# Products with w_in by Strassen's seven multiplications, and layer one for all tokens before layer two

## What is computed

```python
def _moe_ref(x, w_in, w_out, s, b):
    h = x @ w_in
    r = np.maximum(h, 0.0)
    g = s * (r * r) + b
    return g @ w_out

def _moe2_ref(x, w_in, w_out, alpha):
    h = x @ w_in
    g = np.maximum(h, 0.0) + alpha * np.minimum(h, 0.0)
    return g @ w_out
```

## Time and profile before

| | |
|---|---|
| median of 3 timed runs | 1099.71 us (1098.87 to 1099.93) |
| span of the profiled execution | 1098.9 us; nothing shows its own time apart from that |
| matmuls | 4867, of which 4608 in the steps |
| TensorE busy (PE) | 1086.0 us |
| VectorE busy (DVE) | 635.3 us |
| ScalarE busy (ACT) | 592.0 us |
| GpSimd busy (POOL) | 14.6 us |
| moved by DMA | 33.44 MB |

### The profile page before, as it was taken

How to read it: one execution, slowest core, us unless ns; L and a number is a source line. 1 busy time by engine, 2 the same in 40 slices (tenths; PEclk the granted TensorE clock), 3 DMA queues, 4 the chain that set the end, 5 groups by cost and what they waited for, 6 DMA issues and landing times.

```text
span 1098.9 us, 14358 instructions
## 1 busy us (share of the span) xinstructions
PE 1086.0 (99%) x4867; PEld 909.9 (83%) x4867; DVE 635.3 (58%) x980; ACT 592.0 (54%) x1073; POOL 14.6 (1%) x19
## 2 busy tenths in 40 slices
PE   8899999999999999999999999999999999999998
PEld 6788888888888888888888888888888888889887
DVE  6877755645645645655555555564564564565554
ACT  5565646446546546545545644644654654654654
POOL 1110000000000000000000000000000000000000
PEclk9999999999999999999999999999999999999999
DMA  9632201101101001011010010110110000001010
GB/s 356 228 96 77 58 1 20 20 1 20 20 0 19 7 12 19 0 19 19 0 19 15 4 19 0 19 19 0 19 19 0 14 7 12 1 1 20 1 20 16
DMA packets 106719, 33.44 MB, mean 30 GB/s; under 512 B 98480, under 2 KB 103104, under 8 KB 106176
## 3 DMA queue, kind: packets, MB, share of 16 engines
q1 hardware_dynamic: 106560, 33.04, 12.0%
q0 software_dynamic: 128, 0.01, 0.0%
HBM read 26.88 MB, written 6.16 MB: 30 GB/s over the span
## 4 chain that ended last, share of the span: by engine, by line
PE 98%; DMA 1%; DVE 0%; SPq 0%; ACT 0%; issue 0%; DVEq 0%
PE acc L375 16%; PE hid L375 16%; PE acc L377 16%; PE hid L377 16%; PE acc L376 16%; PE hid L376 16%; PE acc L438 4%; DMA qk_raw<-in_k_dram 1%; PE hid L480 0%; PE hid L485 0%; PE hid L481 0%; SPq L289 0%; PE acc L480 0%; PE acc L481 0%; PE acc L485 0%; DVE logit L754 0%
## 5 line engine op out<-in xcount | busy, mean ns | idle before, releaser
L555 ACT ACTIVATE pos<-hid 128x512 f32<-128x512 f32 (+1 forms) x384 | 225.3, 587 | 265.0 <-PE hid L377 263.2
L375 PE MATMUL acc<-act_hi,wo_hi 128*128 128x512 f32 (+1 forms) x768 | 295.5, 385 | 0.0
L377 PE MATMUL acc<-act_hi,wo_lo 128*128 128x512 f32 (+1 forms) x768 | 295.3, 385 | 0.0
L376 PE MATMUL acc<-act_lo,wo_hi 128*128 128x512 f32 (+1 forms) x768 | 295.3, 385 | 0.0
L700 DVE SCALAR_TENSOR_TENSOR act<-neg,nalpha,pos 128x512 f32<-128x512 f32 (+1 forms) x192 | 142.2, 741 | 235.0 <-ACT pos L555 235.0
L678 DVE TENSOR_TENSOR act_lo<-act,act_hi 128x512 fp32r<-128x512 f32 (+1 forms) x384 | 258.4, 673 | 0.1
L697 DVE TENSOR_TENSOR act<-pos 128x512 f32<-128x512 f32 (+1 forms) x192 | 130.4, 679 | 200.9 <-ACT pos L555 199.5
L533 ACT ACTIVATE act_hi<-act 128x512 fp32r<-128x512 f32 (+1 forms) x384 | 237.8, 619 | 0.3 <-DVE act L700 0.3
L554 ACT ACTIVATE neg<-hid 128x512 f32<-128x512 f32 (+1 forms) x192 | 113.2, 589 | 203.9 <-PE hid L377 203.9
L375 PEld LDWEIGHTS acc<-act_hi,wo_hi 128*128 128x128 f32 x768 | 144.2, 188 | 27.9 <-DVE act_lo L678 0.5
L376 PEld LDWEIGHTS acc<-act_lo,wo_hi 128*128 128x128 f32 x768 | 144.2, 188 | 27.4
(11 more groups left out here) (101 smaller groups left out, 556.1 us busy)
## 6 DMA issues: line engine op xcount, KB each, us to landing
v_raw<-in_v_dram SPq DMA_DIRECT2D x44, 128.0 KB, 3.3
out_dram<-y_sq SPq DMA_DIRECT2D x44, 128.0 KB, 2.5
qk_raw<-in_q_dram SPq DMA_DIRECT2D x10, 512.0 KB, 11.2
qk_raw<-in_k_dram SPq DMA_DIRECT2D x10, 512.0 KB, 12.2
stage<-in_moe_w_in_dram SPq DMA_DIRECT2D x4, 1024.0 KB, 9.1
stage<-in_moe_w_out_dram SPq DMA_DIRECT2D x4, 1024.0 KB, 5.4
qk_raw<-in_q_dram SPq DMA_DIRECT2D x1, 384.0 KB, 12.1
qk_raw<-in_k_dram SPq DMA_DIRECT2D x1, 384.0 KB, 13.5
```

What stands on the lines that cost most here:

```text
L375: pe.matmul(dst, w_hi, x_hi, start=start, stop=False)
L376: pe.matmul(dst, w_hi, x_lo, start=False, stop=False)
L377: return pe.matmul(dst, w_lo, x_hi, start=False, stop=stop)
L555: sc.activation(pos[:, f % 2, 0:w], hid[:, f % 2, 0:w], ACT.Relu).then_inc(relu_done, 1)
```

## The change

Tokens now go in pairs of tiles, five pairs of 2 x 512 and one of 2 x 448. For a pair, hidden units (two halves of 1024), channels (two blocks of 128) and tokens (two tiles) make a 2 x 2 by 2 x 2 product of blocks, and that is made by Winograd's form of Strassen's scheme: seven products in place of eight. One of 8 steps j handles 128 units of either half, that is four blocks of hidden (C11, C12, C21, C22).

- Weights: `ws_hi` and `ws_lo` hold for each j the four blocks of w_in and the sums S1 to S4 in seven slots. For layer one DVE (first half) and POOL (second half) make the sums before the steps; for layer two POOL makes them during the last pair of layer one, and ACT and DVE split them then (`ws_high`, `ws_low`, `wo_high`, `wo_low`: the swap, steps 40 to 49 of 96). Only one layer's weights lie in SBUF.
- Tokens: POOL makes the four sums of a pair's blocks (`x_sums`) and all seven low parts (`x_low`), ACT the seven high parts (`x_high`), during the pair before.
- PE makes seven products a step into four banks, three of them accumulating onto an earlier one. ACT copies product 1 out of PSUM (`copy_m1`), DVE adds it up with others (`sum_u2`, `sum_u3`, `sum_c22`, `sum_c21`, `sum_c12`); C11 is a bank of PSUM as it stands. Then relu, gate and split as before, layer one's squares of C22 and C11 on ACT. `project` is unchanged in number: 24 matmuls a step.
- Layer one runs for all six pairs and stores its output to `x2_dram` in DRAM; then layer two loads it (`load_x`) pair by pair. A pair's output goes through three slots `ev`.
- Everything is unrolled. q and k have 7 load slots in place of 8.

The core of the diff:

```diff
+TILE = 512
+PAIRS = 6
+LAST_TILE = (N - (PAIRS - 1) * 2 * TILE) // 2
+STEPS = NF // 2
+PROD = 7
+RUNS = 2 * PAIRS
...
+A11, S2, S3, S1, A12, A22, S4 = range(PROD)
+
+C11, C12, C21, C22 = range(4)
+
+X_ORDER = (0, 4, 6, 1, 3, 2, 5)
...
+    x2_dram = nc.dram_tensor("x2_dram", (PAIRS, 2, CB, P, TILE), F32, kind="Internal").ap()
...
+        SWAP = (PAIRS - 1) * STEPS
+
+        def ws_step(i):
+
+            return i // 2 if i < STEPS else SWAP + i - STEPS + 1
+
+        def wo_step(i):
+            return i - 1 if i < STEPS else SWAP + i - STEPS + 2
...
+            for run in range(RUNS):
+                for j in range(STEPS):
+                    n = run * STEPS + j
+                    if j == 0 and run + 1 < PAIRS:
+                        load_v(run + 1, 0)
+                    if j == 0 and PAIRS <= run + 1 < RUNS:
+                        load_x(run + 1)
+                    if run == 0 and j + 2 < STEPS:
+                        load_wo(j + 2)
+                    if n in (SWAP, SWAP + 1):
+                        load_wo(STEPS + n - SWAP)
+                    if 3 <= n - SWAP <= STEPS:
+                        load_wo(STEPS + n - SWAP - 1)
+                    if 0 <= n - SWAP < STEPS:
+                        load_w2(n - SWAP)
+                    if j == 0 and run > 0:
+                        for t in range(2):
+                            for b in range(CB):
+                                store(run - 1, t, b)
+                    if j == 1 and run + 1 < PAIRS:
+                        load_v(run + 1, 1)
...
+            def x_sums(run):
+
+                w = width(run)
+                if layer(run) == 0:
+                    pool.wait_ge(v_turned, 2 * CB * (run + 1))
+                else:
+                    pool.wait_ge(x_loaded, 64 * (run - PAIRS + 1))
+                x = [xf[:, s, 0:w] for s in range(PROD + 1)]
+                link(pool.tensor_tensor(x[3], x[B12], x[0], ALU.subtract))
+                link(pool.tensor_tensor(x[1], x[6], x[3], ALU.subtract))
+                pool.tensor_tensor(x[2], x[B12], x[6], ALU.subtract)
+                pool.tensor_tensor(x[5], x[4], x[1], ALU.subtract).then_inc(t_ready, 1)
+
+            def x_low(run, i):
+                s, w = X_ORDER[i], width(run)
+                pool.wait_ge(x_hi_done, PROD * run + i + 1)
+                pool.tensor_tensor(x_lo[run % 2][:, s, 0:w], xf[:, s, 0:w], f32(x_hi[run % 2][:, s, 0:w]),
+                                   ALU.subtract).then_inc(x_split, 1)
...
+                    for i in range(1, STEPS):
+                        if n == ws_step(i):
+                            ws_low(i)
+                    if run == 0:
+                        add_wsum(j)
+                    if 0 <= n - SWAP < STEPS:
+                        pool.wait_ge(w2_loaded, 64 * (n - SWAP + 1))
+                        merge(lambda s: w2_tmp[:, s, :])
+                    if run + 1 < RUNS:
+                        if j == 3:
+                            x_sums(run + 1)
+                        for i in {4: (0, 1), 5: (2, 3), 6: (4, 5), 7: (6,)}.get(j, ()):
+                            x_low(run + 1, i)
...
+            def product(run, j, s, dst, start):
+                w = width(run)
+                if j == 0:
+                    pe.wait_ge(x_split, PROD * run + X_PLACE[s])
+                if s == 0 and layer(run) == 0 and run == 0:
+                    pe.wait_ge(ws_split, j + 1)
+                if s == 0 and run == PAIRS:
+                    pe.wait_ge(ws_split, STEPS + j + 1)
+                return three_passes(dst[:, 0:w], ws_hi[:, j, s, :], ws_lo[:, j, s, :],
+                                    x_hi[run % 2][:, s, 0:w], x_lo[run % 2][:, s, 0:w], start, not start)
...
+            def step(run, j):
+                n = run * STEPS + j
+                wait(pe, pos_done[C11], n)
+                product(run, j, 0, h_a, True).then_inc(m1_done, 1)
+                wait(pe, u2_done, n)
+                if n == STEPS:
+                    pe.wait_ge(bias2_ready, 1)
+                product(run, j, 1, h_b, True).then_inc(m6_done, 1)
+                if n > 0:
+                    project(*before(n), C11, first=j == 1)
+                    if j == 1:
+                        project(*before(n), C22, first=True)
+                wait(pe, sum_done[C21], n)
+                product(run, j, 2, h_c, True).then_inc(m7_done, 1)
+                wait(pe, sum_done[C12], n)
+                product(run, j, 3, h_d, True).then_inc(m5_done, 1)
+                if n > 0:
+                    project(*before(n), C21, first=False)
+                pe.wait_ge(s1_done, n + 1)
+                product(run, j, 4, h_a, False).then_inc(m2_done, 1)
+                pe.wait_ge(u3_done, n + 1)
+                product(run, j, 5, h_c, False).then_inc(m4_done, 1)
+                if n > 0:
+                    project(*before(n), C12, first=False)
+                pe.wait_ge(sum_done[C22], n + 1)
+                product(run, j, 6, h_d, False).then_inc(m3_done, 1)
+                if j > 0:
+                    project(run, j, C22, first=False)
...
+                copy_m1(run, j)
+                if n > 0:
+                    g_high(n - 1, C12)
+                splits(n)
+                if layer(run) == 0:
+                    positive(run, j, C22)
+                    square(run, j, C22)
+                    positive(run, j, C11)
+                    g_high(n, C22)
+                    square(run, j, C11)
+                    if out_of is not None:
+                        x2_out(out_of, 0)
+                    positive(run, j, C21)
+                    g_high(n, C11)
+                    x_highs(run, j)
+                    g_high(n, C21)
+                    if out_of is not None:
+                        x2_out(out_of, 1)
+                    positive(run, j, C12)
...
+                    negative(run, j, C22)
+                    positive(run, j, C22)
+                    negative(run, j, C11)
+                    g_high(n, C22)
+                    positive(run, j, C11)
+                    if out_of is not None:
+                        x2_out(out_of, 0)
+                    negative(run, j, C21)
+                    positive(run, j, C21)
+                    g_high(n, C11)
+                    x_highs(run, j)
+                    g_high(n, C21)
+                    if out_of is not None:
+                        x2_out(out_of, 1)
+                    negative(run, j, C12)
+                    positive(run, j, C12)
...
+            def sum_u2(run, j):
+                n, w = run * STEPS + j, width(run)
+                ve.wait_ge(s1_done, n + 1)
+                ve.wait_ge(m6_done, n + 1)
+                ve.tensor_tensor(u2[:, 0:w], h_b[:, 0:w], u2[:, 0:w], ALU.add).then_inc(u2_done, 1)
...
+                if n > 0:
+                    gate(n - 1, C12)
+                sum_u2(run, j)
+                if n > 0:
+                    g_low(n - 1, C12)
+                splits(n)
+                sum_u3(run, j)
+                sum_c22(run, j)
+                if layer(run) == 1:
+                    gate(n, C22)
+                if run + 1 < PAIRS and j in (1, 3):
+                    for b in range(CB):
+                        turn_v(run + 1, j // 2, b)
+                sum_c21(run, j)
+                g_low(n, C22)
+                if layer(run) == 1:
+                    gate(n, C11)
+                if j == 0 and run > 0:
+                    pair_out(run - 1, 0)
+                gate(n, C21)
+                g_low(n, C11)
+                sum_c12(run, j)
+                if j == 0 and run > 0:
+                    pair_out(run - 1, 1)
+                if n == STEPS - 1:
+                    ve.wait_ge(colsum_ready, 1)
+                    ve.tensor_scalar(bias2, colsum_ps, scal[:, 2:3], None, ALU.mult).then_inc(bias2_ready, 1)
+                    ve.wait_ge(bias2_ready, 1)
+                g_low(n, C21)
```

More of the change, by code:

```diff
@@ L52, with width, token @@
 assert sum(ROWS_OF) == ROWS
[L53 to L78, removed]
+RAW = 7
+WQ = 512
+QUARTERS = F // WQ
+W_PIECES = [(b, q) for q in (0, 2, 1, 3) for b in range(CB)]
+W1_BLOCKS = ((0, 1, S4), (0, 0, A11), (1, 1, A22), (1, 0, A12))
+EV = 3
+def width(run):
+    return LAST_TILE if run % PAIRS == PAIRS - 1 else TILE
+def token(pair, t):
+    return pair * 2 * TILE + t * width(pair)
 def wait(eng, sem, count):
-    if not isinstance(count, int) or count > 0:
+    if count > 0:
         eng.wait_ge(sem, count)
@@ L356, in _ @@
[L356 to L369 removed]
+            x_sums(0)
@@ new lines, in negative @@
+            def negative(run, j, blk):
+                n, w = run * STEPS + j, width(run)
+                src = source(run, j, blk)
+                if blk == C22:
+                    wait(sc, g_done[C21], n)
+                elif blk == C11:
+                    wait(sc, g_done[C12], n)
+                elif blk == C21:
+                    sc.wait_ge(g_done[C22], n + 1)
+                else:
```

(35 more changed lines are left out.)

853 lines of the change are left out of this document (432 added, 421 removed).

## The result

The changed kernel takes 1182.44 us (median of 4 runs, 1177.55 to 1184.41); the kernel before, on the same chip, takes 1099.49. The ratio is 1.0747, interval 1.0733 to 1.0760: slower by 7.5%, where 1% was forecast, and outside the range of 1066 to 1142.

The account below looks back on a forecast made before the run. PE bounds layer one, DVE and ACT order layer two: 69.5 + 960.1 + 2.5 + 33 + 10.7 + 2 + 11.5 + 1.2 + 4.3 = 1094.8. Adding 0.8 and 15 for collisions: 1110 us, range 1066 to 1142.

Parts of the forecast that it names:

- Matmuls and their spacing: Main steps: 45 matmuls in place of 48, 0.2267 us each at 512 columns, 10.2 us a step; 64.0 us saved.
- The walk round the order: DVE and ACT order in a step: layer two 10.86 us, 33 us given back; layer one 9.41, so PE bound.
- The unknown, POOL beside DVE: POOL's SBUF reads delaying DVE instructions with two SBUF operands: nothing to 41 us, taken as 15.
- The rival with full blocking: POOL holds DVE back fully, from layer two's first step: 1136 us, up to 1142 with ws_low; chance 0.26.
- the bound: Upper end for POOL beside DVE: 33 us in layer two's five runs, 8 in layer one, together 41.
- The row that I weighed against the rule: Profile row: affine_select beside two DVE 256-column instructions taking 0.76 us, DVE unharmed; rule: whoever comes second is blocked.
- (4): Tail: after PE's 1.2 us wait, drain 0.33, transpose 0.6 and store 2.6, about 4.3 us with hops.
- (1): Outputs: layer two's transposes in DVE's order, 9 us for five runs plus 1.7; layer one's output 2 us.
- (2): Weight swap, layer one's last run and two steps of layer two: 1.3 us a step for 7 steps, then 2.5: 11.5.
- (3): Prologue: first step starts near 69.5, 1.5 us lost; POOL's other sums and ws split cost 2.5 us more.
- PE bound in both layers: Faster rival: layer two's round is 10.2 us or less instead of 10.86, giving 1058 us; chance 0.16.
- Square: Rival: Square on ACT needs table loads, 120 us at two a layer-one step; with other recurring waits over 1145, chance 0.10.

Follow-up runs that it names:

- e1: Changed kernel with POOL's sums, low parts of tokens and weights and w_out running sum replaced by memsets of the same outputs: 1114.28 us.
- e7: Changed kernel with POOL's token work and layer one's ws_low on DVE, seven output slots, C12's gate later, splits behind sum_c22: 1095.57 us.
- e4: Changed kernel with copy of M1 and sum_u2 ahead of C12's signs and gate, g_low of C12 behind sum_c22: 1138.91 us.

## Why the prediction was wrong

**Matmuls and their spacing: right.** 4579 instructions in all as counted, 45 a step, 10.2 us; layer one's quiet steps show it.

**The walk round the order: right.** 10.86 forecast, 10.91 measured in layer two; 9.41 for layer one, so PE bound at 10.2, measured 10.20. The gap of PE is in front of C22's first matmul, ended by g_lo, as said; the trace's 0.40 us of idle is less than the 0.5 to 0.7 named.

**The unknown, POOL beside DVE: the step that failed.** I took 15 us, between 0 and 41 (47 with ws_low); e1 shows 68. Two errors lie in it. The first is the choice in the range: the argument that POOL would mostly be the one to wait has no support in the trace, where both wait: DVE's gates go to 1.6 to 1.8 us, POOL's instructions to 1.5 to 1.6. The rival with full blocking had the mechanism, and in layer two its size was near, 26 us for 33. In layer one it was too small: the bound had 1.3 us a run, and the four quiet runs lost 12.4, some 3.1 each. The second error is that the bound had next to nothing for what stands outside these runs, 6.5 + 11.6 + 11.3 = 29.4 us: DVE's own S sums beside the tokens' first low parts (1.63 to 1.77 us, not 0.69), the first run with POOL's weights and wsum, and the run that reads weights, where merge joins x_low. Of these only 6 us for ws_low and 1.3 for each of the two runs stood in the range. The row that I weighed against the rule speaks for it: there POOL was the one that waited. The same affine_select begins at 6.07 in the changed kernel, takes 0.31 in place of 0.56, and ends at the same 0.15 us behind DVE's second sum. Nor was that row the only one: in the kernel before, win_lo (L684) starts at 54.89 beside POOL's L353 and lasts 0.68, but POOL ends 0.09 later, so it decides nothing.

The prologue shows this second error in two rows of the changed kernel:

```profile
64.71 5.07 POOL L382 TENSOR_TENSOR x_lo<-xf,x_hi 128x512 fp32r<-128x512 f32 x3
65.22 1.77 DVE L970 TENSOR_TENSOR w_tmp<-w_tmp 128x512 f32<-128x512 f32 x1
```

**The remaining 17 us** (e1's span of 1112.1 against the sum of 1094.8) are edges. (4) The tail was forecast at 4.3 us after the last matmul; from its end at 1168.12 to the end of the span it is 11.6, so 7.3 were missing. I took the store of one tile (2.64) from the kernel before, where only that was left; here four tiles leave in 16 stores, one after another. The span of before also ends 2.15 us behind its last store, which the sum did not carry. From the last copy of M1 (1154.61) to the end of the last matmul it is 13.5 us, where a step of 9.84 and 1.2 were walked: 2.5 more at least. (1) Outputs of layer two: e1 has 24.5 to 24.6 us for the two steps where 23.5 was forecast, and the last run, where a store is late for its slot, is 4.2 over; some 9 in all. (2) The swap was forecast at 9 for the run itself and is 10.5 without POOL's reading: near. Against these, the first step began some 2 us earlier in e1 than walked and its first run is 3 us shorter, since the memsets are quick. The small rest is about what the quiet steps add, 10.91 for 10.86 in layer two and 9.12 for 9.0 with 448 columns in layer one. (3) That the first step of the changed kernel began at 73.67, not 69.5, belongs to the collisions: in e7, where POOL does not read beside DVE there, it begins at 70.04.

**Rivals.** PE bound in both layers (1058) is what e4's order gives in the quiet steps, by a change of order that was not made. Square needed no table load: the changed kernel has two, as the kernel before. Two of the forecast's own signs of being wrong came true: the gates average over 0.8 us (0.879 and 0.964), and PE's granted clock falls at the gaps (below).

## What to carry to other kernels

Before work goes to an idle POOL, count the DVE instructions with two SBUF operands that it will stand beside, in every stretch, the prologue and the rare runs too, and price each meeting at the rest of POOL's instruction; here 0.68 us of work on DVE was cheaper than 1.53 us on POOL. Such a delay costs only where the chain has no slack, so the order is worked out first: ahead of each engine's next product stands what releases another engine, and splits come last. Two remedies for one chain are not added; run them together before believing their sum.

## What the runs showed of the hardware

TensorE's granted clock falls around short gaps of PE. Windows around the gap of 4.09 us (columns: window, length, busy time of PE, PEld, DVE, ACT and POOL, granted clock, DMA share, GB/s):

```profile
801.10:809.00 7.90, 3.64 (x16) 2.37 (x14) 7.76 (x9) 3.90 (x8) 6.29 (x4) 0.96 0.14 25
809.00:812.00 3.00, 3.00 (x8) 2.38 (x9) 2.86 (x5) 1.63 (x3) 0.00 (x0) 0.53 0.53 93
812.00:815.00 3.00, 3.00 (x15) 2.46 (x14) 2.33 (x5) 0.63 (x1) 0.00 (x0) 1.00 0.60 104
```

Around a PE gap of 4.09 us the clock is at the lower level (1.2 GHz), from 808.4 to 811.8, and matmuls start 0.42 to 0.43 us apart instead of 0.2267: 8 in 3 us, then 15. Up to its last matmul the changed kernel has nine such stretches from the first step on, 41 us in all, and e1 has one, of 7 us; the kernel before had none between 147 and 1053 us.

They cost time of their own, and this can be read from the trace. The second steps of two runs of layer two, the fourth and the fifth, have no POOL work, the same instructions and the same wait of DVE for an output slot (1.2 us):

```profile
904.38:919.18 14.80, 13.48 (x49) 10.74 (x49) 9.88 (x15) 7.34 (x15) 0.00 (x0) 0.78 0.32 55
1000.92:1013.82 12.90, 12.38 (x52) 9.73 (x51) 9.93 (x15) 7.35 (x14) 0.00 (x0) 0.92 0.36 63
```

With the granted clock at 0.78 the step takes 14.80 us, at 0.92 it takes 12.90. In the longer one DVE waits 1.74 and 0.38 us for PE, in the other not at all:

```profile
910.17 0.69 DVE L812 TENSOR_TENSOR cb<-hcd,u 128x512 f32<-128x512 f32 x1 [1.74 <-PE hcd L435]
```

So a part of the 68 us is the clock's, by way of the gaps that POOL's reading makes. How large it is over the whole kernel was not tried; the forecast named the falling clock as a sign of being wrong, but had no term for it.
